# Attention decays prepared in another way: inverse squares by ScalarE, and the next batch's preparation in thirds

## What is computed

```python
# q, k, v, a: batch 4, heads 8, seq 768, head_dim 48
mag = sqrt(a_re*a_re + a_im*a_im)
scale = minimum(mag, 0.999) / (mag + 1e-6)
a = a * scale                      # complex, |a| just under 1
for t in range(768):               # state S: 48 x 48 complex per head
    S = a[t][:, None] * S + outer(k[t], v[t])
    y[t] = q[t] @ S.re
x = y in rows of 3072 tokens x 384
# 1: soft mixture: logits = x @ phi, softmax over tokens and over slots,
#    8 experts with w1, w2 and a relu;  2: relu(x @ w_in)**2 @ w_out
```

## Time and profile before

| what | us |
|---|---|
| median of 3 runs | 667.14 (663.59 to 668.21) |
| the profiled execution | 665.93 |
| its span, first to last instruction | 664.2 |
| DVE busy, whole span | 425.3 (64%) |
| PE busy, whole span | 518.4 (78%) |
| ACT busy, whole span | 324.6 (49%) |
| POOL waited for the product steps (its memsets) | 267.5 |

### The profile page before, as it was taken

How to read it: one execution, slowest core, us unless ns; L and a number is a source line. 1 busy time by engine, 2 the same in 40 slices (tenths; PEclk the granted TensorE clock), 3 DMA queues, 4 the chain that set the end, 5 groups by cost and what they waited for, 6 DMA issues and landing times.

```text
span 664.2 us, 11659 instructions
## 1 busy us (share of the span) xinstructions
PE 518.4 (78%) x4537; PEld 394.2 (59%) x4537; DVE 425.3 (64%) x680; ACT 324.6 (49%) x563; POOL 147.1 (22%) x128
## 2 busy tenths in 40 slices
PE   2000049796497967998798988899999999999997
PEld 1000026575375655776587863457888888888886
DVE  4799998979969999999653215049932323332332
ACT  5774135383555746333143431157655656555653
POOL 6001000100001000010000000016755555555553
PEclk9999978798797998999898999899999999999999
DMA  6400084734935534588898899900010101010011
GB/s 253 142 1 0 3 221 97 150 81 89 246 62 120 132 74 97 120 262 240 163 228 186 219 422 424 437 29 1 1 48 0 49 0 48 0 49 1 6 43 47
DMA packets 40022, 79.59 MB, mean 120 GB/s; under 512 B 7200, under 2 KB 28832, under 8 KB 38048
## 3 DMA queue, kind: packets, MB, share of 16 engines
q1 hardware_dynamic: 36224, 62.33, 33.8%
q10 hardware_dynamic: 3744, 16.52, 7.9%
HBM read 55.12 MB, written 4.72 MB: 90 GB/s over the span
## 4 chain that ended last, share of the span: by engine, by line
PE 55%; DVE 20%; DMA 8%; issue 7%; SPq 5%; ACT 5%; DVEq 0%; ACTq 0%
PE ps L1306 9%; PE ps L1302 9%; PE ps L1303 9%; PE ps L1036 9%; DMA stk<-xout 8%; SPq L261 4%; PE ps L1276 3%; DVE big L704 3%; DVE xout L825 2%; PE ps L1196 2%; PE ps L1022 2%; PE ps L1218 2%; DVE big L693 2%; PE ps L1076 2%; DVE big L734 1%
## 5 line engine op out<-in xcount | busy, mean ns | idle before, releaser
L1001 DVE TENSOR_TENSOR qs<-rs 128x512 f32<-128x512 f32 x96 | 81.0, 844 | 119.4 <-ACT rs L590 119.4
L660 POOL TENSOR_TENSOR hlo<-qs,hhi 128x512 fp32r<-128x512 f32 x96 | 126.4, 1317 | 130.9 <-DVE qs L1001 127.4
L1036 PE MATMUL ps<-stk 112*128 112x224 f32 (+1 forms) x384 | 92.7, 407 | 49.2 <-DMA stk<-xout 49.0
L1022 PE MATMUL ps<-ident 128*32 128x512 bf16 x245 | 71.7, 395 | 69.0 <-DVE xout L825 69.0
L1036 PEld LDWEIGHTS ps<-stk 112*128 112x128 f32 x384 | 81.7, 235 | 61.6 <-DMA stk<-xout 55.6
L1302 PE MATMUL ps<-hhi,who 128*128 128x512 f32 x285 | 110.9, 389 | 0.0
L1303 PE MATMUL ps<-hhi,wlo 128*128 128x512 f32 x285 | 110.9, 389 | 0.0
L590 ACT ACTIVATE rs<-ps 128x512 f32<-128x512 f32 x96 | 57.4, 598 | 82.1 <-PE ps L1276 81.9
L1306 PE MATMUL ps<-hlo,who 128*128 128x512 f32 x285 | 80.5, 391 | 0.1
L1022 PEld LDWEIGHTS ps<-ident 128*32 128x32 bf16 x245 | 19.4, 97 | 89.7 <-DVE xout L825 69.3
L647 POOL MEMSET big<- 128x2304 f32 x4 | 8.2, 2038 | 267.5 <-DVE big L734 267.5
(11 more groups left out here) (163 smaller groups left out, 820.2 us busy)
## 6 DMA issues: line engine op xcount, KB each, us to landing
stk<-xout SPq DMA_DIRECT2D x144, 128.0 KB, 3.9
wt<-in_w SPq DMA_DIRECT2D x10, 1536.0 KB, 17.2
xq<-in_xq SPq DMA_DIRECT2D x24, 384.0 KB, 4.8
big<-in_a_all ACTq DMA_DIRECT2D x9, 768.0 KB, 4.9
vr<-in_v_all SPq DMA_DIRECT2D x24, 192.0 KB, 4.1
wt<-in_w ACTq DMA_DIRECT2D x3, 1536.0 KB, 8.0
wt<-in_w ACTq DMA_DIRECT2D x6, 768.0 KB, 7.6
out<-ost SPq DMA_DIRECT2D x5, 768.0 KB, 3.5
```

What stands on the lines that cost most here:

```text
L660: pool.tensor_tensor(hlo[:, i % NHS, :], qs[:, i % NQS, :], hhi[:, i % NHS, :].bitcast(F32), ALU.subtract).then_inc(lo_ready, 1)
L1001: dve.tensor_tensor(qs[:, i % NQS, :], rs[:, i % NQS, :], rs[:, i % NQS, :], ALU.mult).then_inc(sq_ready, 1)
L1022: nc.tensor.matmul(ps[P - SL:P, bank, :], idb[:, 0:SL], idle, start=True, stop=True)
L1036: last = nc.tensor.matmul(ps[:, h // 2, h % 2 * SK:h % 2 * SK + cols], x[:, 0:CH], x[:, CH:CH + cols], start=True, stop=True)
```

## The change

- The inverse squares come from the products themselves. ScalarE squares real and imaginary part (product_squares: first the blocks 0 to 2, "part 0", then block 3, "part 1"), DVE adds them (square_sums), ScalarE takes logarithm and exponential (inverse_squares). norm_squares, scaled_mag, end_norms, inverses and GpSimd's memsets go. The order in M_ changes with it, and weigh reads it with other strides.
- weigh waits for m_ready alone, and stands behind the first key_query.
- The table `parts` has other costs, so that parts of the products fall into other half chunks.
- SyncE: stack_turns of a batch stands behind the last chunk's restack instead of ahead of it.
- ScalarE: the preparation of the next batch (squares at c = 1, root and overshoot at c = 2, logarithm at c = 3) is split by thirds t = 0, 1, 2: ahead of the kts copies, behind them, and behind the st copy.

```diff
-            def norm_squares(b):
-
-                act.wait_ge(sm_ready, DT * (b + 1))
...
+            def product_squares(b, part, c):
+
+
+                act.wait_ge(chain, C_ALL * b + (C_BLOCK if part else C_BLOCK - 7))
+                if b >= 2 and part == 0:
+                    act.wait_ge(weighed, NC * (b - 1))
+                x, dims = PART[part]
+                o = N_ if c else M_[b % 2]
+                nc.scalar.activation(grid(o + x, *dims), grid(PL[b % 2] + c * PF + x, *dims), ACT.Square).then_inc(m_squares, 1)
+
+            def inverse_squares(b):
+                for part in range(2):
+                    act.wait_ge(chain, C_ALL * b + C_BLOCK + part + 1)
+                    x, dims = PART[part]
+                    m = grid(M_[b % 2] + x, *dims)
+                    nc.scalar.activation(m, m, ACT.Ln).then_inc(m_log, 1)
+                act.wait_ge(m_log, 2 * (b + 1))
+                m = grid(M_[b % 2], [1, PF])
+                nc.scalar.activation(m, m, ACT.Exp, scale=-1.0).then_inc(m_ready, 1)
...
+                    if c == NC - 1 and p < B:
+                        product_squares(p, 1, 0)
+                        product_squares(p, 1, 1)
...
                     if 0 <= n < NT and has_turn(n):
                         copy_kt(n, 1)
+                    if p < B - 1 and c < NC - 2:
+                        prepare(p + 1, c, 1)
+                    if p < B and c == NC - 2:
+                        product_squares(p, 0, 0)
+                    if c == NC - 1 and p < B:
+                        inverse_squares(p)
                     if c == NC - 1 and p < B - 1:
                         signs(p + 1)
...
                     if 0 <= n < NT and has_turn(n):
                         copy_state(n)
+                    if p < B - 1 and c < NC - 2:
+                        prepare(p + 1, c, 2)
+                    if p < B and c == NC - 2:
+                        product_squares(p, 0, 1)
...
-                    if c == NC - 2 and p < B:
+                    if c == NC - 1 and p < B:
                         stack_turns(p)
...
+            def square_sums(b, part):
+                dve.wait_ge(m_squares, 4 * b + 2 * part + 2)
+                x, dims = PART[part]
+                m = grid(M_[b % 2] + x, *dims)
+                dve.tensor_tensor(m, m, grid(N_ + x, *dims), ALU.add).then_inc(chain, 1)
...
-            parts = [4] + [14] * (BL - 1) + [48] * (NB4 - 1) + [8, 18, 52]
+            parts = [4] + [14] * (BL - 1) + [48] * (NB4 - 1) + [20, 9, 18]
...
                     if 0 <= n < NT:
+                        key_query(n, 0)
                         weigh(n)
-                        key_query(n, 0)
                         key_query(n, 1)
```

More of the change, by code:

```diff
@@ L76, in program @@
         tt = place("tt", [P, 3, BW])
-        esq = place("esq", [P, 3, TF, NC], offset=tt_at)
-        tu = place("tu", [P, 6, DT, NC - 1], offset=tt_at + 4 * 4 * TF * NC)
+        tu = place("tu", [P, 6, DT, NC - 1], offset=tt_at)
         xout = place("xout", [P, NOUT, 2, DT, 2 * CH])
@@ L205, in program @@
         C_BLOCK = C_SCAN + 7 * (NB4 - 1)
-        C_END = C_BLOCK + 3
-        C_TURN = C_END + 10
-        C_ALL = C_TURN + 1
+        C_END = C_BLOCK + 2
+        C_ALL = C_END + 10
+        BC = BL * NC
+        PART = [(0, ([HP, TF], [1, (NB4 - 1) * BC])), ((NB4 - 1) * BC, ([HP, TF], [1, BC]))]
         def turns(n):
@@ L264, in stack_turns @@
             def stack_turns(b):
-                sp.wait_ge(chain, C_ALL * b + C_TURN)
+                sp.wait_ge(chain, C_ALL * (b + 1))
                 if b:
@@ L507, in _ @@
                     if p < B - 1:
[L508 to L520, removed]
+                        prepare(p + 1, c, 0)
+                        if c == NC - 2:
+                            prepare(p + 1, c, 1)
+                            prepare(p + 1, c, 2)
                     pair = pair_at(n)
@@ L642, in _ @@
             assert made[0] == NCONST
[L644 to L649, removed]
             pool.wait_ge(y_done, NT)
@@ L771, in turn_factors @@
                 n1 = NC - 1
+                dve.wait_ge(chain, C_ALL * b + C_BLOCK)
                 if b:
@@ L816, in key_query @@
                     dve.wait_ge(weighed, n + 1)
-                elif n >= NOUT:
-                    k = n - NOUT
-                    dve.wait_ge(stacked[k % NST], 96 * (k // NST + 1))
+                else:
+                    dve.wait_ge(chain, C_ALL * (b + 1))
+                    dve.wait_ge(ld_xq[n % NXQ], 16 * (n // NXQ + 1))
+                    if n >= NOUT:
+                        k = n - NOUT
+                        dve.wait_ge(stacked[k % NST], 96 * (k // NST + 1))
                 e = grid(PL[b % 2] + 2 * c, [HP, 2 * TF], [2 * NC, HC // 2], [1, 2])
@@ L864, in part @@
                     block_step(b, k - BL + 1)
-                elif k == BL + NB4 - 1:
-                    end_norms(b)
-                elif k == BL + NB4:
+                elif k < BL + NB4 + 1:
+                    square_sums(b, k - BL - NB4 + 1)
+                else:
                     turn_factors(b)
-                else:
-                    inverses(b)
             def parts_in(b, lo, hi):
@@ L889, in _ @@
                 normalise(0, t)
-            for t in range(DT):
-                scaled_mag(0, t)
             dve.wait_ge(consts, NCONST)
@@ L923, in _ @@
                             norm2(p + 1, t)
-                    if p < B - 1 and c == NC - 1:
-                        for t in range(DT):
-                            scaled_mag(p + 1, t)
             running_max(NT // 2 - 1)
```

55 lines of the change are left out of this document (18 added, 37 removed).

## The result

The changed kernel takes 676.01 us (median of 4 runs, 674.83 to 678.25), the kernel before on the same chip 665.74 (also four runs; the 667.14 given ahead of the prediction was over three of them). The ratio is 1.0157, with a 95% interval of 1.0108 to 1.0206: slower, by some 10 us. The profiled execution took 676.21 us, its span is 674.5 us.

What follows compares the result with a forecast made beforehand. DVE was taken to bound passes 1 to 3, also standing in a ring with TensorE and ScalarE. Chunk 12's pair 1.9 us later plus 8.2 gave +10.1: 676.0 profiled, 677 as median, range 661 to 686.

Steps and rivals of the forecast that it cites:

- The start: Pass 0: three scaled_mag, scan and reciprocal go, two adds come, net 5.7 us per batch; chunk 0's pair 6.7 us earlier.
- Down to the mask of chunk 0: From chunk 0's pair to its mask: raw decays' loads now beside the restack; 5.0 us kept, between 6.7 and 3.4.
- the restack would pass the loads: By queues taking turns packet by packet, SyncE's restack passes ScalarE's loads: chunk 0 keeps 6.7, chunk 6 wins 1.2: 674.
- Pass 1, the thirds: Norm2's last third waits behind chunk 1's st copy: norm2 11.2 us behind chunk 0's mask, before 6.5; 4.7 lost.
- The rest of the passes: Passes 1 and 2 after the thirds: batch-end saving of 5.7 us minus a moved step and adds' waits; won 1.5, 1.1.
- Pass 2, the thirds: Norm2 waits for squares behind chunk 7's st copy, ending at 202.9 instead of 198.2, with mask at 187.8; 4.8 us lost.
- The loose end: Chunk 6's restack in pass 2, with raw decays' loads falling 3 us later against it: from 1.2 better to 3.4 worse.
- Pass 3: End of pass 3: DVE waits for ScalarE's squares, logarithm and exponential behind chunk 16's st copy; 9.4 us lost.
- The tail: From pass 3's loss to the end: last restack goes at once, TensorE starts slower; 8.2 of the 9.4 remain, 1.2 won.
- No drain at a table load: ScalarE's table switches cost the 1.28 us load without the page's 1.38 us drain, which would add 2.8 us.
- the ring: DVE masks chunk n, TensorE then scores n+1, ScalarE copies, and DVE's next instruction may wait behind that copy.
- The rival in which the squares come in time: DVE stays the bound and squares come in time: 668, or 646 if pass 3's imaginary square does too; chance 0.2.

Runs made afterwards that it cites:

- e5: Changed kernel, with SyncE issuing the next raw decays' loads behind the restack of a pass's first chunk, instead of ScalarE with the signs: 668.82 us, ratio 1.0067.
- e9: Kernel before, with only the raw decays' loads issued by SyncE behind the restack of a pass's first chunk: 652.15 us, ratio 0.9803.
- e1: Changed kernel, with all three thirds of the next batch's squares ahead of the kts copies at c = 1: 666.94 us, ratio 1.0042.
- e2: Kernel before, with only the preparation split by thirds as in the change (overshoot stays with the logarithm at c = 3): 670.23 us, ratio 1.0102.
- e6: Changed kernel, all four product_squares behind the kts copies at c = 4, and pass 3's inverse_squares right behind chunk 16's st copy: 671.76 us, ratio 1.01.
- e7: Changed kernel, with the edits of e1 and e6 together: 660.9 us, ratio 0.9952 against the kernel before.
- e3: Kernel before, with only SyncE's order changed, stack_turns behind the last chunk's restack: 662.72 us, ratio 0.9977.
- e8: Changed kernel, with the edits of e1, e5 and e6 together: 644.25 us, ratio 0.9678 against the kernel before.
- e10: Kernel before, with the edits of e9 and e3 together: 652.27 us, ratio 0.9785.
- e4: Changed kernel, with part 0's imaginary square right behind the real one, ahead of the xts and st copies: 675.4 us, ratio 1.017 against the kernel before.
- e11: Changed kernel, with the edits of e1 and e5 together: 647.72 us, ratio 0.9715 against the kernel before.

## Why the prediction was right

It said 677.0 us, the result is 676.0; for the profiled execution 676.0, and it took 676.2. The 677 stood on a median before of 667.14, which is 665.74 with the fourth run; as a difference it said 9.9 to 10.1 us, and 10.3 came. By its own steps:

- **The start: 6.7 won, 6.65 measured** (pair 0 at 79.56 for 86.21). The adds cost 1.96 and 0.76, the squares 1.64, the Exp 2.12, and weigh did not wait in pass 0. The signs, priced at 1.3 us for the next init_products, cost nothing there, and 1.25 and 0.86 us at the ends of passes 1 and 2.
- **Down to the mask of chunk 0: 5.0 forecast, 3.1 measured** (101.45 for 104.53), just under the 3.4 that I gave for loads that drain first. The sum took the middle, and that term was mis-sized: the scores started 14.3 us behind the pair for 10.7, since the restack landed after 8.4 us for 6.9, and the last of its six transfers after 10.6 for 7.1 (the median is 3.5 where it meets no load, in e5). The Trainium skill (DMA: Bandwidth & Descriptors, Queues, rings and completion order) has the engines take turns between queues by packets. The trace agrees with that only in part: from 83 to 87 us the queues moved 315 and 259 packets, but for the 3.4 us before that the restack was issued and moved none (1.0 us in e5). What I made of the rule beside the sum, that the restack would pass the loads (674), did not come.
- **Pass 1, the thirds: norm2 11.2 us behind the mask, measured 11.2.** Pair 2 is 1.7 us behind before instead of 0.3 ahead, by the term above.
- **The rest of the passes: 1.5 and 1.1 won, measured 2.8 and 2.4** (pair 2 to 6 and 8 to 12). The first add waited 1.7 us and not 2.5 to 3. That mis-sized term cancelled part of the next.
- **Pass 2, the thirds: norm2 15.2 us behind the mask, measured 15.2.** The loose end, which the sum put at nothing, went the wrong way: chunk 6's mask came 22.7 us behind its pair for 19.0, 3.7 us more, just outside the +3.4 that I gave as its worst. Of these, 2.7 are the later start of the scores and 1.0 the 16 matmuls (6.34 us for 5.30). Pair 12 is 5.2 us behind instead of 1.9.
- **Pass 3: 9.4 lost, measured 7.7.** The chain from the st copy to the pair is 12.1 us for 11.9, the waits 4.63 and 3.93 for "about 5" and "some 4". But the copy came 0.9 us earlier against pair 12, where I had put it 1.0 later. Pair 18 is 12.9 us behind for 11.3.
- **The tail: 1.2 won, measured 2.6** (12.9 at pair 18, 10.3 at the end). In e9, whose edit leaves this stretch alone, it differs from the kernel before by 3.3 us, so the tail is not measured better than that.
- **No drain at a table load**, as taken from the earlier trace rows. The Trainium skill (ScalarE: Activation LUTs, What ACT_TABLE_LOAD costs) has 1.38 us for one; the measured Ln starts 1.29 us behind the load's start, and by the page pass 3 would have been 2.8 us longer.

So the mechanism stood, with the waits where and about as long as forecast. That the total came within 0.2 us is luck: two terms were 2.0 and 3.9 us too good (the two restacks) and four were 1.3 to 1.7 us too bad (the rest of passes 1 and 2, pass 3, the tail), and they cancelled.

The opening reading was the weaker part. I took DVE for the bound with the ring beside it. That holds in pass 3, but e9 shows that in passes 1 and 2 of the kernel before some 11 us lay in the restacks that met the loads, with DVE's work left alone. Of the loss, the thirds are shown by e1 and e2. The squares and logarithms on copies are shown by e6 and e7: another 3.8 us from the changed kernel, or 6.0 from e1. The last restack first, for which I allowed nothing to pay, cost nothing that e3 could find.

The rival in which the squares come in time priced that at 668, and at 646 for its far end, where the first add also waits for nothing. e7 makes the squares early with the transfers as they were: 660.9. e8's 644 is not that far end, since some 14 of its 21 us come from the transfers, which e10 has without the change. The 5.7 us of a batch that I summed up for DVE were there in full at the start alone; from e9 to e8, pass 1 gave 4.3, pass 2 gave 2.2, and pass 3 took 5.1 back.

## What to carry to other kernels

Before moving work off the busiest engine, look whom it will wait for in its new queue. In ScalarE's queue an instruction behind a copy that TensorE releases started only when TensorE was done, however short the queue ahead (e4); put it ahead of the wait that would leave the engine idle (e11). A busy share of some 90% does not exclude a second bound (91% and 89% in passes 1 and 2, where e9 won 11 us; at 98%, in pass 3, it won nothing). When everything hangs in one ring, ask for each transfer of the ring what else uses the DMA engines at that moment. Do not add up gains measured alone: the loads' edit gave 6 us where the thirds held norm2, 13 in the kernel before and 22 where nothing else did (e1 to e11).

## What the runs showed of the hardware that was not expected

- Six transfers of 128 KB landed in 3.5 us each (median, e5) where they met no load, and in 6.9 us (before) and 8.4 us (changed) behind and beside loads of 768 KB on another queue. Their first packet came 3.4 us behind the first issue instead of 1.0. What held it so long, while packets of the other queue went on, stays open. The three loads, sent behind the restack instead, took a median of 6.7 us to land, for 8.5 in the changed kernel.
- TensorE's 16 matmuls of a chunk's scores take 3.29 us behind other work, and also behind waits of 1.43 us (e9) and 2.04 us. Behind 1.70 us (e3) they took 4.98, behind 4.1 to 11.8 us between 4.85 (e5) and 6.34 (e8), in no order of the wait's length. Passes 1 and 2 of the changed kernel have a mean granted clock of 0.85, those of e8 0.92 and 0.90. A late restack can so cost up to 3 us more than its wait; what decides between 3.29 and 4.98 at about 2 us stays open.
- Chunk 17's scores, 16 matmuls of 128 columns, took 2.05 us at 326.00 for 3.48 at 324.53 in the earlier trace rows, behind waits of 1.29 and 4.17 us.
